# Attention stage of a fused attention and MoE kernel: in each period TensorE turns the probabilities before it forms the values

## What is computed

```python
def _attn_ref(q, k, v, n_sink, window):          # q, k, v: 2 x 8 x 768 x 64
    scores = scale * np.matmul(q, k.transpose(0, 1, 3, 2))
    pos = np.arange(S)
    is_sink = pos[None, :] < int(n_sink)         # 4 sinks
    rel = pos[:, None] - pos[None, :]
    in_window = (rel >= 0) & (rel < int(window)) # window of 128
    keep = is_sink | in_window
    scores = np.where(keep, scores, -1000000000.0)
    scores = scores - np.max(scores, axis=-1, keepdims=True)
    a = np.exp(scores)
    a = a / (np.sum(a, axis=-1, keepdims=True) + 1e-09)
    return np.matmul(a, v)
```

## Time and profile before

| | |
|---|---|
| time, median of three runs | 852.86 us |
| span of the profiled execution, first to last instruction | 851.0 us |
| its share of TensorE, busy | 842.8 us, 99% |
| DVE, ScalarE, GpSimd busy | 605.4, 401.6, 172.1 us |
| 60 us of attention, mean of a triple of periods: TensorE | 9.87 of 9.87 us busy |
| the same for ScalarE, DVE, GpSimd | 9.12, 8.52, 7.63 us |
| granted clock of TensorE | 1.00 in all of these stretches, and over the span |

### The profile page before, as it was taken

One profiled execution on the slowest core, in us unless ns is written; L12 is line 12 of the kernel. 1 busy time (PEld: TensorE's weight loads), 2 busy tenths in 40 slices (PEclk: granted clock), 3 DMA queues, 4 the chain that ended last, 5 costly groups with the idle time before them and its releaser, 6 DMA issues.

```text
span 851.0 us, 13888 instructions
## 1 busy us (share of the span) xinstructions
PE 842.8 (99%) x4518; PEld 729.6 (86%) x4518; DVE 605.4 (71%) x1170; ACT 401.6 (47%) x739; POOL 172.1 (20%) x259
## 2 busy tenths in 40 slices
PE   7999999999999999999999999999999999999998
PEld 5777888888888888898999899889989998999897
DVE  7888799898888989876566565565565555656655
ACT  6999754448754549754324314314414413422410
POOL 6778200001100112222012112102202202202100
PEclk9999999999999999999999999999999999999999
DMA  7555730004830006825045135225225315403304
GB/s 257 143 162 154 159 100 1 1 0 97 194 106 0 0 0 127 162 59 115 19 104 117 28 89 117 43 74 117 56 61 117 68 49 117 92 25 68 69 0 151
DMA packets 25622, 72.70 MB, mean 85 GB/s; under 512 B 4336, under 2 KB 6512, under 8 KB 25584
## 3 DMA queue, kind: packets, MB, share of 16 engines
q0 software_dynamic: 10720, 33.82, 22.1%
q1 hardware_dynamic: 14576, 38.04, 13.1%
q10 hardware_dynamic: 288, 0.39, 0.1%
HBM read 35.28 MB, written 3.15 MB: 45 GB/s over the span
## 4 chain that ended last, share of the span: by engine, by line
PE 99%; DMA 0%; POOL 0%; DVE 0%; ACT 0%; issue 0%; SPq 0%; DVEq 0%
PE banks L944 31%; PE banks L870 28%; PE banks L839 15%; PE banks L636 15%; PE banks L651 3%; PE banks L732 3%; PE banks L702 3%; PE banks L738 1%; DMA pool<-kT 0%; POOL pool L480 0%; PE banks L705 0%; PE banks L957 0%; ACT pool L1067 0%; DVE pool L1863 0%; DVE pool L1486 0%
## 5 line engine op out<-in xcount | busy, mean ns | idle before, releaser
L1789 DVE SCALAR_TENSOR_TENSOR pool<-banks,p_norm,pool 128x512 f32<-128x512 f32 x179 | 132.8, 748 | 66.1 <-PE banks L944 64.3
L944 PE MATMUL banks<-w_hi,g_lo 128*128 128x512 f32 x382 | 149.9, 392 | 0.0
L944 PE MATMUL banks<-w_lo,g_hi 128*128 128x512 f32 x382 | 149.7, 392 | 0.0
L944 PE MATMUL banks<-w_hi,g_hi 128*128 128x512 f32 x382 | 148.7, 389 | 0.0
L1291 ACT ACTIVATE g_hi<-pool 128x384 fp32r<-128x384 f32 x96 | 50.5, 526 | 190.7 <-DVE pool L1769 139.1
L870 PE MATMUL banks<-x_hi,w_lo 128*128 128x384 f32 x256 | 86.0, 336 | 0.0
L870 PE MATMUL banks<-x_hi,w_hi 128*128 128x384 f32 x256 | 85.9, 335 | 0.0
L870 PE MATMUL banks<-x_lo,w_hi 128*128 128x384 f32 x256 | 85.7, 335 | 0.0
L944 PEld LDWEIGHTS banks<-w_hi,g_lo 128*128 128x128 f32 x382 | 71.7, 188 | 15.0
L944 PEld LDWEIGHTS banks<-w_hi,g_hi 128*128 128x128 f32 x382 | 71.7, 188 | 13.8 <-issue 0.2
L944 PEld LDWEIGHTS banks<-w_lo,g_hi 128*128 128x128 f32 x382 | 71.7, 188 | 13.8
(11 more groups left out here) (151 smaller groups left out, 1776.3 us busy)
## 6 DMA issues: line engine op xcount, KB each, us to landing
w_raw<-weights SPq DMA_DIRECT2D x48, 512.0 KB, 4.4
w_lo<-w_raw POOLq DMA_DIRECT2D x48, 512.0 KB, 5.5
w_lo<-w_sum POOLq DMA_DIRECT2D x15, 384.0 KB, 4.0
pool<-v SPq DMA_DIRECT2D x8, 384.0 KB, 3.5
out<-pool SPq DMA_DIRECT2D x11, 256.0 KB, 2.0
pool<-kT SPq DMA_DIRECT2D x7, 400.0 KB, 5.0
pool<-qT SPq DMA_DIRECT2D x7, 384.0 KB, 4.1
w_lo<-pool POOLq DMA_DIRECT2D x2, 384.0 KB, 4.9
```

Source lines behind the costliest of these rows:

```text
L944: mm = pe.matmul(banks[:, bank, :], g[:, s, f * SUP + at:f * SUP + at + P], w_cols(w, p2 * SLOT + DOWN_AT[f], DM), start=(f == 0 and n == ...
L1789: dve.scalar_tensor_tensor(out=to, in0=d_bank, scalar=share, in1=to, op0=ALU.mult, op1=ALU.add)\
```

## The change

In each period the turn now stands ahead of the values. Nothing else is edited, and the tail after the last period keeps its order (values ahead of turns).

```diff
                 def period(ct, g, before):
                     scores(ct, g)
+                    if at := group_at(ct, g, TURN_LAG, before):
+                        turn(*at)
                     if at := group_at(ct, g, VALUES_LAG, before):
                         values(*at)
-                    if at := group_at(ct, g, TURN_LAG, before):
-                        turn(*at)
```

## The result

The changed kernel takes **855.62 us** (median of six runs, 855.51 to 855.80), the kernel before 852.82 us beside it; the ratio is 1.0034 with a 95% interval of 1.0022 to 1.0045. It is slower by 2.80 us, and the prediction had 2.96. The profiled execution has a span of 853.7 us, against 851.0.

The account below looks back on a forecast made before the run. TensorE, busy 99% of the span, was taken as the bound. Waits for DVE's take 1.92, GpSimd 0.2, the opening 0.67 and a shape change 0.17 sum to 2.96 us: 852.86 becomes 855.8 us, range 853.7 to 857.3.

Parts of the forecast that it names:

- What bounds: Whole span: TensorE is busy 99%, so a wait on it costs its full length to the program's end.
- The take's term: Six loop turns: the eighth transpose waits for DVE's take, 0.23 to 0.39 us each, 1.92 us in all.
- Rival 2: Attention stage: earlier copies pull DVE's masks, take and inversion forward, shrinking the first wait; 853.9 us, chance 0.17.
- GpSimd's term: Six other loop turns: the eighth transpose waits for GpSimd's gathering copy, 0.04 us each, 0.2 us in all.
- The opening: First moved turn, period 3: its fifth transpose waits for GpSimd's second half of group 1, 0.67 us.
- Change of shape: TensorE's array shapes: still three changes a period, one more at the stage's end, before the networks; +0.17 us.
- Rival 3: Attention stage: turn to values costs no shape change, saving up to 2.9 us; 850.5 to 851 without waits; chance 0.04.
- The sum: Whole kernel: all waits plus the extra shape change add 2.96 us, giving 855.8 us.
- Rival 4: Attention stage: late weight loads make each of 13 waits cost 0.1 to 0.2 us more; 857.5 us, chance 0.14.

Follow-up runs that it names:

- e4: Kernel before, with the turn ahead of the values only in period 3, the opening: 853.39 us, ratio 1.0007.
- e2: Kernel before, with the turn ahead of the values only in periods 4, 7, ..., 22, whose turn waits for GpSimd: 855.07 us, ratio 1.0027.
- e5: Changed kernel, with DVE's take moved ahead of the period's two first masks: 857.07 us, ratio 1.0050 to the kernel before.
- e6: Changed kernel, with DVE's take moved behind the inversion: 857.59 us, ratio 1.0056 to the kernel before.
- e3: Kernel before, with the turn ahead of the values only in periods 5, 8, ..., 23, whose turn has neither wait: 852.90 us, ratio 1.0002.
- e1: Kernel before, with the turn ahead of the values only in periods 6, 9, ..., 21, whose turn waits for DVE's take: 854.38 us, ratio 1.0019.
- e7: Changed kernel, with DVE's take and inversion behind the first mask in the loop, second mask after them: 854.45 us, ratio 1.0020 to the kernel before.

## Why the prediction was right

- **What bounds.** TensorE at 99%, and a wait on it kept to the end: 2.82 us at 81 us of the span are 2.7 to 2.8 at its end. Shown by the traces and by e4.
- **The take's term.** Foreseen 0.39, 0.30, 0.38, 0.23, 0.39, 0.23 (1.92 us); measured, in this order, 0.34, 0.25, 0.33, 0.17, 0.33, 0.17: 1.6 us. The pattern is right to the turn, each is 0.05 to 0.06 too long. The reason is in the trace: I took the lateness of the weight load for the length that the block gains, and the block gains 0.05 less. T7's eighth weights came 34.77-33.76=1.01 into the turn, due at 0.71, so 0.30 late as foreseen; the block is 0.25 longer. That the mask stays 0.94 behind the scores was the doubtful step, and it holds: 30.46-29.52. (DVE isn't busy without a gap from there to the take, as I had it: in period 8 it stands idle for 0.2 ahead of the take of a first half, at 32.68 here and as long before, so nothing changes by it.) Rival 2, the chain that moves forward with the turn, fell there; its own terms make 854.0 and not 853.9, and with 0.1 for each of six waits 854.3.
- **GpSimd's term.** Foreseen 0.04 six times (0.2 us) behind the gathering copy; measured 0.08 six times, 0.46. The term was mis-sized because I put the wait on the eighth transpose. The fifth wants GpSimd's last product too: from the earlier trace rows, 34.05+2.43=36.48, with the semaphore 8.05 after S8, and TensorE is there at 4.24+1.13+0.30+0.81+1.12+0.38=7.98, 0.07 late. TensorE was there another 0.05 earlier, because T7 waited 0.25 and not 0.30, so the weights were 0.12 late, as the trace has them (37.58 against 37.46), and the block is 0.08 longer. The gathering copy costs nothing: it makes the eighth weights 0.02 late, and their product is on time. That both terms hang on one chain, so that one grows where the other goes, is what e2, e5 and e6 show.
- **The opening.** 0.67 foreseen, 0.62 measured, alone and in the changed kernel: the weights are 0.67 late, and it is the same 0.05.
- **Change of shape.** 0.17 foreseen at the end, 0.17 measured, in T21 (e3 and the changed kernel). Three changes a period cost the same in either order: S to T, T to V and V to S have the lengths of S to V, V to T and T to S. Rival 3 fell with that. The even pace into the sink's transpose was read rightly: turn to values, with the sink's transpose between them, still shows the 0.20 of a change (34.94 to 35.15). The Trainium skill, page "TensorEngine Tiling (Array Packing)", Tiling Modes, has the rule that a change of mode drains the array. e3's trace agrees in that no order of the three was free: each change shows as 0.20 from a turn's or values' last start to the next block, where the transposes follow each other in 0.11. The 128x64 mode of its list doesn't show as one that the sink's transpose shares with the values here.
- **The sum.** 1.60 + 0.46 + 0.62 + 0.17, less 0.04 that V6 lost before and doesn't now: 2.81, against 2.82 at the first product and 2.80 in the time. That 855.8 is this close is luck: the take's and the opening's terms were 0.37 us too large together, GpSimd's was 0.26 too small.
- **Rival 4**, dearer waits: the scores behind a wait were not late, and the values waited for no copy. Its slower step behind a wait is real, below, but the load's lead over its product outweighs it.

## What to carry to other kernels

On an engine that is full, a step moved forward is paid for in the slack of what it needs. Measure that slack from the event that starts the other engines' chain, not from the step's neighbours: here the scores' start, 5.2 us ahead of the take's end. Two waits on one chain are not a sum; take the first away and the second grows, so look for the chain and shorten that. And exchange only those instances of a step that have the slack: a third of the turns could move for nothing but the 0.17 us at the stage's end.

## What the runs showed that I had not expected

- A late weight load costs TensorE 0.05 us less than it is late, in every turn that came out longer, in the changed kernel and in e1 to e7 (0.04 to 0.05). By the starts of T7's single instructions, a load stands 0.105 ahead of its product. Behind a wait the product starts together with its weights (1.016 into the turn), which takes 0.105 off; the next transpose then follows in 0.166 instead of 0.109, which puts 0.057 back. In e7 the loads of eleven turns are 0.12 to 0.14 late, and the turns 0.07 to 0.09 longer.
- PE's busy time rose by 1.7 us (844.5 against 842.8) with the same 4518 instructions: short waits count as busy there.
- DVE's steps don't keep their spacing when they are exchanged (e5: 1.54 us instead of 1.35 for the same four).
